# The first MLP of an attention and two-MLP kernel as 48 steps of one tile's up product and another's down share, with one attention unit in a step and the log1p remainder moved to VectorE

## The chip, the cores and the metric

The kernel runs on one core of a Trainium2 chip. A core has TensorE (matmuls, PE in the profile), VectorE (DVE), ScalarE (ACT), GpSimd (POOL) and SyncE (SP, which here only issues transfers), each with an instruction queue of its own that runs in order; they meet at semaphores. The metric is the device time of one execution in microseconds, as the median of several runs.

## What is computed

Window attention (each row sees itself and the 63 before it), then an MLP with a softplus, then four gated experts with a ReLU. All is in float32.

```python
# q, k, v: (2, 8, 576, 64); x becomes (1152, 512) after attention
scores = np.where(mask, scale * q @ k.T, -1e9)           # mask: 0 <= row - col < 64
attn = softmax(scores) @ v
h = x @ w_in                                             # (1152, 2048)
g = np.maximum(h, 0.0) + np.log1p(np.exp(-np.abs(h)))
x = g @ w_out                                            # (1152, 512)
p = domain_probs / (domain_probs.sum(-1, keepdims=True) + 1e-09)
for e in range(4):
    out += p[:, e:e+1] * (np.maximum(x @ w1[e], 0.0) @ w2[e])
```

## The kernel before

**Numbers.** Every float32 operand of the MLPs is split into a high part in float32r and a low part, `wa` (up weights), `wb` (down weights), `xy` (the input) and `hid` (the hidden values) each exist as `[0]` high and `[1]` low, and each product is three matmuls (`TERMS`). So a tile's up product (128 hidden rows by 384 tokens, four k tiles) is 12 matmuls of 128x384, and its down share (four output tiles `t`) is 12 more.

**First MLP.** The 1152 tokens are 3 chunks `c` of 384, the 2048 hidden columns 2 blocks `b` of 8 tiles `f`. A loop over n = 0 to 5 (b = n // 3, c = n % 3) does in each turn 20 stages: eight up products (`up`, L698), then the down products in 12 pieces of 2 or 3 tiles (`down_width`, L713, `PIECES`). Both use the four PSUM banks `ps[0]` to `ps[3]`: up tile f writes bank f % 4, the down sum of output tile t stands in bank t. So up tile f + 4 waits until VectorE has read tile f's bank (`bank_read`), the down sum waits for the last four tiles, and the next turn's up waits for the sums' copies (`down_read`).

**Softplus of a tile.** ScalarE: `absolute` (L381), `exponential` (L386), `logarithm` (L393, log(1+e) into `sp_l`). VectorE: `rounded` (L501, (e + 1) - 1 into `sp_c`), GpSimd: `lost` (L299, e - `sp_c`, the remainder that the logarithm lost), VectorE: `relu_ln` (L507, reads the bank, frees it), `activation` (L515, adds the remainder). Then ScalarE `hidden_high` (L398) and VectorE `hidden_low` (L520) give the two parts of `hid`.

**Attention.** 24 units u of 192 rows by 2 heads, 8 to a chunk. A unit passes `scores` (TensorE L650), `masked_scores` (VectorE L467), `softmax_exp` (ScalarE L349), `row_inverse` (VectorE L474, L476), `normalise` (GpSimd L292), `transpose_probs` (L661), `copy_pT` (ScalarE L358), `weigh_values` (L676), `x_high` (ScalarE L365), `x_low` (VectorE L482). Units 0 to 7 run ahead of the MLP in a prologue of 11 turns j, with the first pieces of up products between them (`STARTS`, `BEFORE`); units 8 to 23 run in the turns n = 0 and 1 behind the stages in `AFTER`. The queries, keys and values of two units are a group g = u // 2, in one of four slots.

**Splits and transfers.** The raw weights come in pairs of tiles into two buffers (`raw_a` up, `raw_b` down). SyncE issues all transfers in one order; the third and later pairs of a block wait until both splits of the pair before the last are done (L213, L214 and L220, L221). In block 0 VectorE makes the high parts (L578, L602) and GpSimd the low ones (L313, L326), at stages given by `UP_SPLIT` and `DOWN_SPLIT`; afterwards ScalarE and VectorE do (L339, L450; L344, L455), except the down weights of block 1, which are VectorE's and GpSimd's too. `first_out` (L528, L530) takes the down sums to `part`, and `y_high` and `y_low` split them for the experts, which start at 286.38 us in the profiled execution (L698 and L728).

## Time and profile before

| | us |
|---|---|
| median of 3 runs (lowest to highest) | 687.87 (685.45 to 688.37) |
| span of the profiled execution | 686.2 |
| TensorE busy | 654.9 |
| VectorE busy | 319.0 |
| ScalarE busy | 224.8 |
| GpSimd busy | 119.4 |
| start of the experts in the profiled execution | 286.38 |

The span is the time from the first to the last instruction of the one execution that was profiled. An engine's busy time is a sum of what its instructions took, in which a wait for a shared resource inside an instruction counts as busy. Matmuls overlap: one takes 0.33 us and the next starts 0.17 us after it, so the pace is read from starts and not from durations.

### The profile page before, as it was taken

How to read it: one execution, taken by the hardware profiler on the slowest of the kernel's cores; microseconds unless marked ns; L12 is line 12 of the kernel's file. 1: busy time of each engine (PE TensorE's matmuls, PEld its weight loads, DVE VectorE, ACT ScalarE, POOL GpSimd, SP SyncE). 2: the span in 40 equal slices, each digit the busy share in tenths (PEclk: the TensorE clock that was granted, in tenths of full speed). 3: DMA queues.
4: the chain of work that ended last, by engine and by line, in shares of the span. 5: the costliest groups of instructions: out<-in, count | busy, mean ns of one | idle time of the engine just before them, and what ended most of it. 6: DMA issues, size and time to landing. Idle time of an engine off the chain costs nothing.

```text
span 686.2 us, 10024 instructions
## 1 busy us (share of the span) xinstructions
PE 654.9 (95%) x3688; PEld 603.9 (88%) x3688; DVE 319.0 (46%) x689; ACT 224.8 (33%) x565; POOL 119.4 (17%) x111
## 2 busy tenths in 40 slices
PE   7886998999969999999999999999999999999998
PEld 6776998898959898998999999898989898989896
DVE  5599369376793939651224232133322142512121
ACT  4655556564531627440112221121311030402020
POOL 3676334231452415000000000000000000000000
PEclk9999999999999999999999999999999999999999
DMA  7662520103030000330003130002120030100101
GB/s 205 195 151 94 138 63 1 51 1 107 22 117 1 0 1 1 123 123 0 1 2 120 22 103 0 1 31 91 47 75 0 0 101 22 61 31 15 38 8 46
DMA packets 39425, 37.94 MB, mean 55 GB/s; under 512 B 12256, under 2 KB 32096, under 8 KB 39392
## 3 DMA queue, kind: packets, MB, share of 16 engines
q1 hardware_dynamic: 39392, 37.51, 18.3%
q8 instruction: 19, 0.31, 0.2%
q14 instruction: 14, 0.11, 0.1%
HBM read 35.15 MB, written 2.36 MB: 55 GB/s over the span
## 4 chain that ended last, share of the span: by engine, by line
PE 71%; DVE 14%; issue 7%; DMA 3%; ACT 2%; SPq 2%; POOL 1%; DVEq 0%; ACTq 0%
PE ps L698 33%; PE ps L728 29%; PE ps L713 6%; DVE sp_l L515 4%; DVE sp_l L507 3%; DVE hid_lo L520 3%; DMA raw_a<-in_w_in 2%; PE ps_o L676 1%; DVE wa_lo L450 1%; SPq L191 1%; DVE prob L467 1%; DVE sp_c L501 1%; ACT prob L349 1%; PE ps_pT L661 1%; ACT sp_l L393 1%
## 5 line engine op out<-in xcount | busy, mean ns | idle before, releaser
L698 PE MATMUL ps<-xy_hi,wa_hi 128*128 128x384 f32 (+1 forms) x576 | 194.2, 337 | 4.5 <-DVE sp_l L507 3.7
L698 PE MATMUL ps<-xy_hi,wa_lo 128*128 128x384 f32 (+1 forms) x576 | 192.8, 335 | 0.0
L698 PE MATMUL ps<-xy_lo,wa_hi 128*128 128x384 f32 (+1 forms) x576 | 192.8, 335 | 0.0
L427 ACT ACTIVATE hid_hi<-ps 128x384 fp32r<-128x384 f32 x96 | 47.3, 492 | 304.1 <-PE ps L698 304.1
L698 PEld LDWEIGHTS ps<-xy_hi,wa_hi 128*128 128x128 f32 x576 | 108.2, 188 | 7.5 <-issue 6.0
L728 PE MATMUL ps<-wb_hi,hid_lo 128*128 128x512 f32 x288 | 112.3, 390 | 0.0
L728 PE MATMUL ps<-wb_lo,hid_hi 128*128 128x512 f32 x288 | 112.2, 390 | 0.0
L728 PE MATMUL ps<-wb_hi,hid_hi 128*128 128x512 f32 x288 | 112.0, 389 | 0.0
L698 PEld LDWEIGHTS ps<-xy_lo,wa_hi 128*128 128x128 f32 x576 | 108.3, 188 | 0.4
L698 PEld LDWEIGHTS ps<-xy_hi,wa_lo 128*128 128x128 f32 x576 | 108.2, 188 | 0.0
L614 DVE SCALAR_TENSOR_TENSOR hid_lo<-ps,hid_hi 128x384 fp32r<-128x384 f32 x96 | 53.5, 558 | 116.0 <-ACT hid_hi L427 116.0
L632 DVE SCALAR_TENSOR_TENSOR part<-ps,gate,part 128x512 f32<-128x512 f32 x36 | 27.0, 751 | 161.0 <-PE ps L728 161.0
L713 PE MATMUL ps<-hid_hi,wb_hi 128*128 128x384 f32 x192 | 68.4, 356 | 14.1 <-DVE sp_l L507 11.5
L299 POOL TENSOR_TENSOR sp_c<-sp_e,sp_c 128x384 f32<-128x384 f32 x48 | 59.9, 1249 | 95.1 <-DVE sp_c L501 95.1
L713 PE MATMUL ps<-hid_hi,wb_lo 128*128 128x384 f32 x192 | 65.0, 339 | 0.0
L713 PE MATMUL ps<-hid_lo,wb_hi 128*128 128x384 f32 x192 | 64.9, 338 | 0.0
L728 PEld LDWEIGHTS ps<-wb_hi,hid_lo 128*128 128x128 f32 x288 | 54.1, 188 | 11.3
L728 PEld LDWEIGHTS ps<-wb_lo,hid_hi 128*128 128x128 f32 x288 | 54.1, 188 | 11.0
L728 PEld LDWEIGHTS ps<-wb_hi,hid_hi 128*128 128x128 f32 x288 | 54.1, 188 | 10.9
L520 DVE TENSOR_TENSOR hid_lo<-sp_l,hid_hi 128x384 fp32r<-128x384 f32 x48 | 57.5, 1197 | 0.0
L713 PEld LDWEIGHTS ps<-hid_hi,wb_hi 128*128 128x128 f32 x192 | 36.3, 189 | 20.7 <-DVE sp_l L507 16.2
L381 ACT ACTIVATE sp_e<-ps 128x384 f32<-128x384 f32 x48 | 23.5, 489 | 55.1 <-PE ps L698 50.7
(74 smaller groups left out, 625.2 us busy)
## 6 DMA issues: line engine op xcount, KB each, us to landing
raw_a<-in_w SPq DMA_DIRECT2D x16, 512.0 KB, 3.8
raw_b<-in_w SPq DMA_DIRECT2D x16, 512.0 KB, 4.0
raw_a<-in_w_in SPq DMA_DIRECT2D x8, 512.0 KB, 5.1
raw_b<-in_w_out SPq DMA_DIRECT2D x8, 512.0 KB, 4.3
v_in<-in_v SPq DMA_DIRECT2D x20, 192.0 KB, 3.6
k_in<-in_kT SPq DMA_DIRECT2D x9, 256.0 KB, 3.5
out_dram<-part SPq DMA_DIRECT2D x9, 256.0 KB, 2.1
q_in<-in_q SPq DMA_DIRECT2D x22, 96.0 KB, 3.0
```

Of the source, the lines that this page charges most:

```text
L191: sp.dma_start(q_slots[s][D * h:D * h + D, :, :, WIN * h:WIN * h + WIN], q[h, :, u, hp0:hp0 + 2, :, :]).then_inc(qk_in[s], 16)
L299: pool.tensor_tensor(sp_c[:, s, :], sp_e[:, s, :], sp_c[:, s, :], ALU.subtract).then_inc(lost_done, 1)
L381: act.activation(sp_e[:, s, :], ps[f % 4][:, 0:CH], ACT.Abs).then_inc(abs_done, 1)
L427: act.activation(hid[0][:, f, :], ps[f % 4][:, 0:CH], ACT.Relu).then_inc(h_hi, 1)
L507: dve.scalar_tensor_tensor(out=l, in0=ps[f % 4][:, 0:CH], scalar=0.0, in1=l, op0=ALU.max, op1=ALU.add).then_inc(bank_read, 1)
L515: dve.tensor_tensor(l, l, sp_c[:, f % 2, :], ALU.add).then_inc(act_done, 1)
L520: dve.tensor_tensor(hid[1][:, f, :], sp_l[:, (i - 1) % 4, :], f32(hid[0][:, f, :]), ALU.subtract).then_inc(h_lo, 1)
L614: dve.scalar_tensor_tensor(out=hid[1][:, f, :], in0=ps[f % 4][:, 0:CH], scalar=0.0, in1=f32(hid[0][:, f, :]), op0=ALU.max, op1=ALU.subtrac ...
L632: dve.scalar_tensor_tensor(out=acc[:, T, :], in0=ps[t][:, :], scalar=gate[:, T, bass.ds(e, 1)], in1=acc[:, T, :], op0=ALU.mult, op1=ALU.ad ...
L698: m = pe.matmul(ps[f % 4][:, 0:CH], wa[a][:, f, k, :], xy[x][:, bass.ds(c, 1), k, :], start=(k == 0 and i == 0), stop=(k == KT - 1 and i = ...
L713: m = pe.matmul(ps[t][:, 0:CH], wb[a][:, f, P * t:P * t + P], hid[x][:, f, :], start=(f == 0 and i == 0), stop=(f == FT - 1 and i == 2))
L728: m = pe.matmul(ps[t][:, :], hid[x][:, f, P * t:P * t + P], wb[a][:, f, :], start=(f == 0 and i == 0), stop=(f == FT - 1 and i == 2))
```

## The change

The turn of 20 stages is gone. The first MLP is now 48 steps k (`STEPS`; n = k // 8, f = k % 8). A step on TensorE is: the up product of tile k; the transposes of unit k + 8; the scores of unit k + 10; the down share of tile k - 3 (`LAG`) for all four output tiles; the weighing of unit k + 8. The last three down shares stand among the first three up products of expert 0.

The eight PSUM banks are divided anew. The down sums have four of their own (`sums`: `ps[2]`, `ps[3]`, `ps_score[1]`, `ps_o`). The up products have `ps[0]` and `ps[1]` in turn up to step 15, and four (`up_banks`) from step 16 on. From unit 8 on all scores go through `ps_score[0]`, and transposed probabilities and outputs share `ps_pT`, so a unit's transposes wait for `x_low` of the unit before it.

`lost` moves from GpSimd to VectorE. The prologue scores units 8 and 9 too (`SCORED` = 10) and weighs 8 as before; of the early pieces of tile 2, none is left. The low parts of block 0's down weights stay on GpSimd, one in each of the steps 0 to 7; those of block 1 go to ScalarE and VectorE (`split_down`). On SyncE the inputs of group 7 move between the third and the fourth pair of down weights.

```diff
+LAG = 3
+STEPS = NB1 * NCH * FT
+N_UNITS = NCH * UPC
+SCORED = 10
+WEIGHED = 8
+        up_banks = [ps[0], ps[1], ps_score[0], ps_pT]
+        sums = [ps[2], ps[3], ps_score[1], ps_o]
+        def up_bank(k):
+            return up_banks[k % 2 if k < N_UNITS - WEIGHED else k % 4]
...
 # SyncE
-            for g in range(5, 7):
-                attention_inputs(g)
-            down_weights(0, down_in(0), (2, 3))
+            attention_inputs(5)
+            attention_inputs(6)
+            down_weights(0, down_in(0), (2,))
+            attention_inputs(7)
+            down_weights(0, down_in(0), (3,))
             up_weights(1, up_in(1), (0, 1))
-            for g in range(7, 12):
+            for g in range(8, 12):
                 attention_inputs(g)
...
 # GpSimd
-                if j < UPC:
+                if j < SCORED:
                     normalise(j)
...
+            for k in range(N_UNITS - SCORED):
+                if k < FT:
+                    pool.wait_ge(wb_hi, k + 1)
+                    pool.tensor_tensor(wb[1][:, k, :], ...)
+                normalise(k + SCORED)
...
 # ScalarE
+            for k in range(STEPS):
+                n, f = k // FT, k % FT
+                absolute(n, f)
+                if k + WEIGHED < N_UNITS:
+                    copy_pT(k + WEIGHED)
+                exponential(n, f)
+                if k > 0:
+                    hidden_high((k - 1) // FT, (k - 1) % FT)
+                logarithm(n, f)
+                if k + SCORED < N_UNITS:
+                    softmax_exp(k + SCORED)
+                if k + WEIGHED < N_UNITS:
+                    x_high(k + WEIGHED)
...
 # VectorE
+            for k in range(STEPS):
+                n, f = k // FT, k % FT
+                if k + SCORED < N_UNITS:
+                    masked_scores(k + SCORED)
+                rounded(n, f)
+                if k > 0:
+                    hidden_low((k - 1) // FT, (k - 1) % FT)
+                lost(n, f)
+                relu_ln(n, f)
+                if k + SCORED < N_UNITS:
+                    row_inverse(k + SCORED)
+                if k + WEIGHED < N_UNITS:
+                    x_low(k + WEIGHED)
+                activation(n, f)
+                if n >= 1 and f == LAG - 1:
+                    for t in range(KT):
+                        first_out(n - 1, t)
+                if n == 0:
+                    dve.wait_ge(raw_b_in[f // 2 % 2], 16 * (f // 4 + 1))
+                    dve.tensor_copy(wb[0][:, f, :], ...).then_inc(wb_hi, 1)
+                if n % NCH == NCH - 1:
+                    split_up(n // NCH + 1, f)
+                if 0 <= k - (NCH - 1) * FT - LAG - 1 < FT:
+                    split_down(1, k - (NCH - 1) * FT - LAG - 1)
...
 # TensorE
-                if j + 1 < UPC:
+                if j + 1 < SCORED:
                     scores(j + 1)
...
+            for s in range(STEPS):
+                n, f = s // FT, s % FT
...
+                up(up_bank(s), f, c, n < NCH, [k for k in range(KT) if n > 0 or (f, k) not in started])
+                if s + WEIGHED < N_UNITS:
+                    transpose_probs(s + WEIGHED)
+                if s + SCORED < N_UNITS:
+                    scores(s + SCORED)
+                if s >= LAG:
+                    down_width((s - LAG) // FT, (s - LAG) % FT)
+                if s + WEIGHED < N_UNITS:
+                    weigh_values(s + WEIGHED)
```

**First place, TensorE in the prologue, turn j = 7.** Before, behind the weighing of unit 3 (the row with `ps<-probT`) come the transposes of unit 5:

```order
L650 MATMUL ps_score<-part 128x128 x3
L661 MATMUL ps_pT<-ident,prob 128x128 x3
L676 MATMUL ps<-probT,v_in 64x64 x6
L661 MATMUL ps<-ident,prob 128x128 x3
L676 MATMUL ps_o<-probT,v_in 64x64 x6
```

Now:

```order
L650 MATMUL ps_score<-part 128x128 x3
L663 MATMUL ps_pT<-ident,prob 128x128 x3
L678 MATMUL ps<-probT,v_in 64x64 x6
L650 MATMUL ps_score<-k_in,q_in 128x128 x3
L663 MATMUL ps<-ident,prob 128x128 x3
L678 MATMUL ps_o<-probT,v_in 64x64 x6
```

The scores of unit 8 have come in ahead of the transposes of unit 5, and those of unit 9 stand in the same way one turn later.

**Second place, VectorE in the turns or steps without attention.** Before, a tile's row of work in the turn n = 2 (`lost` is on GpSimd, between L501 and L515):

```order
L501 TENSOR_SCALAR sp_c<-sp_e 128x384
L515 TENSOR_TENSOR sp_l<-sp_l,sp_c 128x384
L520 TENSOR_TENSOR hid_lo<-sp_l,hid_hi 128x384
L507 SCALAR_TENSOR_TENSOR sp_l<-ps,sp_l 128x384
```

Now, step 19, with one split of up weights:

```order
L490 TENSOR_SCALAR sp_c<-sp_e 128x384
L515 TENSOR_TENSOR hid_lo<-sp_l,hid_hi 128x384
L496 TENSOR_TENSOR sp_c<-sp_e,sp_c 128x384
L502 SCALAR_TENSOR_TENSOR sp_l<-ps_pT,sp_l 128x384
L510 TENSOR_TENSOR sp_l<-sp_l,sp_c 128x384
L450 TENSOR_TENSOR wa_lo<-raw_a,wa_hi 128x512
```

The row with `sp_c<-sp_e,sp_c` is `lost`, and `activation` (`sp_l<-sp_l,sp_c`) has moved from the next tile's turn to the end of its own.

**Third place, SyncE's queue of transfers, from the last pair of block 0's up weights on.** This stretch is the same before and now but for line numbers; here it is as it stands now:

```order
L226 DMA raw_a<-in_w_in 128x4x256
L233 DMA raw_b<-in_w_out 128x2x512 x2
L258 DMA gate<-in_probs 128x9x4
L202 DMA q_in<-in_q 64x6x64 x2
L205 DMA k_in<-in_kT 128x2x256
```

The queries and keys at its end are group 5's, units 10 and 11. What moved is their use: the scores of unit 10 stood in turn n = 0 behind the first down piece, and stand now in step 0.

## Rows read from the trace of the kernel before

**Rows 1.** The page: busy time and share of each engine.
```profile
PE 654.9 (95%) x3688; PEld 603.9 (88%) x3688; DVE 319.0 (46%) x689; ACT 224.8 (33%) x565; POOL 119.4 (17%) x111
```

**Rows 2.** Stretches (us, busy by engine, PEclk, DMA share, GB/s): first MLP.
```profile
216.14:251.18 35.04, 33.85 (x193) 33.21 (x193) 23.45 (x44) 16.06 (x36) 11.24 (x9) 1.00 0.00 1
...
30.60:286.38 255.78, 234.15 (x1477) 221.43 (x1474) 181.32 (x406) 130.15 (x345) 102.89 (x86) 0.99 0.22 63
```

**Rows 3.** The same view, 20 us of attention beside the MLP, and the experts.
```profile
40.00:60.00 20.00, 14.95 (x84) 13.34 (x84) 19.93 (x37) 11.09 (x29) 13.03 (x12) 1.00 0.27 66
...
300.00:686.00 386.00, 382.91 (x1939) 348.44 (x1937) 112.25 (x181) 71.71 (x144) 1.38 (x1) 1.00 0.12 39
```

**Rows 4.** Who waited for whom, TensorE (us in total, times, longest).
```profile
PE ps L713 <- DVE sp_l L507: 11.5, 13, 2.0
```

**Rows 5.** The chain of waits (start us, us, what): TensorE at its pace.
```profile
74.01 0.67 PE ps_score L650 x6
...
77.29 0.67 PE ps_score L650 x6
...
216.14 6.25 PE ps L698 x36
```

**Rows 6.** Timeline (start us, us, instruction, idle): GpSimd and VectorE, 45 us.
```profile
45.38 1.32 POOL L299 TENSOR_TENSOR sp_c<-sp_e,sp_c 128x384 f32<-128x384 f32 x1
...
43.59 0.41 DVE L602 CAST wb_hi<-raw_b 128x512 fp32r<-128x512 f32 x1
...
45.75 1.36 DVE L520 TENSOR_TENSOR hid_lo<-sp_l,hid_hi 128x384 fp32r<-128x384 f32 x1
47.03 0.55 DVE L507 SCALAR_TENSOR_TENSOR sp_l<-ps,sp_l 128x384 f32<-128x384 f32 x1
47.50 0.34 DVE L501 TENSOR_SCALAR sp_c<-sp_e 128x384 f32<-128x384 f32 x1
47.77 0.55 DVE L515 TENSOR_TENSOR sp_l<-sp_l,sp_c 128x384 f32<-128x384 f32 x1
```

**Rows 7.** Groups of equal instructions, VectorE, 0 to 310 us.
```profile
L467 DVE CUSTOM_DVE_ANT_0 prob<-ps_score,mask 128x128 f32<-128x128 f32 x72 | 16.9, 285 | 4.9 <-PE ps_score L650 3.6 <-PE ps L661 0.8 <-PE ps_pT L661 0.6
...
L482 DVE TENSOR_TENSOR xy_lo<-ps_o,xy_hi 128x192 fp32r<-128x192 f32 x21 | 7.5, 357 | 16.8 <-ACT xy_hi L365 16.7
...
L474 DVE TENSOR_SCALAR rowsum<-rowsum 128x3 f32<-128x3 f32 x24 | 5.5, 231 | 13.1 <-ACT prob L349 13.1
```

**Rows 8.** The same for GpSimd and ScalarE.
```profile
L326 POOL TENSOR_TENSOR wb_lo<-raw_b,wb_hi 128x512 fp32r<-128x512 f32 x16 | 21.8, 1367 | 13.0 <-DVE wb_hi L602 13.0
L292 POOL TENSOR_TENSOR prob<-prob,rinv 128x384 f32<-128x384 f32 x24 | 21.0, 873 | 38.5 <-DVE rinv L476 38.5
...
L349 ACT ACTIVATE prob<-prob,negmax 128x128 f32<-128x128 f32 x72 | 28.0, 391 | 19.6 <-DVE negmax L467 19.6
```

**Rows 9.** Timeline of TensorE before the first MLP.
```profile
22.79 0.67 PE L661 MATMUL ps<-ident,prob 128*128 128x128 f32 x3 [1.33 <-POOL prob L292]
23.39 0.91 PE L676 MATMUL ps_o<-probT,v_in 128*64 128x64 f32 x12
```

**Rows 10.** Timeline of the transfer queue of SyncE.
```profile
24.17 0.62 SPq L194 DMA_DIRECT2D k_in<-in_kT  x1
...
29.38 0.37 SPq L215 DMA_DIRECT2D raw_a<-in_w_in  x1
...
34.10 1.78 SPq L194 DMA_DIRECT2D k_in<-in_kT  x1
```

**Rows 11.** Issue to landing of the k transfers issued at 24.17 and at 34.10.
```profile
DMA to landing us min/median/max: 4.4/4.4/4.4
...
DMA to landing us min/median/max: 5.9/5.9/5.9
```

**Rows 12.** Timeline of GpSimd: the split that frees a buffer.
```profile
28.03 1.27 POOL L313 TENSOR_TENSOR wa_lo<-raw_a,wa_hi 128x512 fp32r<-128x512 f32 x1 [0.89 <-DVE wa_hi L578]
```

**Rows 13.** A stretch of 1 us at TensorE's lower clock.
```profile
69.00:70.00 1.00, 1.00 (x4) 1.00 (x4) 0.08 (x1) 1.00 (x6) 0.06 (x1) 0.50 0.62 141
```

More of the change, by code:

```diff
@@ L111, in o_bank @@
         def o_bank(u):
+            if u >= UPC:
+                return ps_pT
             return ps[2] if u < N_ALT and u % 2 else ps_o
@@ new lines, in _ @@
+            for k in range(STEPS):
[17 more added lines that the diff above has]
+                    dve.wait_ge(raw_b_in[f // 2 % 2], 16 * (f // 4 + 1))
+                    dve.tensor_copy(wb[0][:, f, :], raw_b[:, f // 2 % 2, f % 2, :]).then_inc(wb_hi, 1)
+                if n % NCH == NCH - 1:
+                    split_up(n // NCH + 1, f)
+                if 0 <= k - (NCH - 1) * FT - LAG - 1 < FT:
+                    split_down(1, k - (NCH - 1) * FT - LAG - 1)
+                for m in range(NCH, NB1 * NCH):
+                    if 0 <= k - FT * (m + 1) - LAG < KT:
+                        y_low(m, k - FT * (m + 1) - LAG)
+                if k == NCH * FT:
@@ L610, in _ @@
                     gates()
+            hidden_low(NB1 * NCH - 1, FT - 1)
             def relu_low(n, f):
                 dve.wait_ge(h_hi, h_count(n, f))
-                dve.scalar_tensor_tensor(out=hid[1][:, f, :], in0=ps[f % 4][:, 0:CH], scalar=0.0,
+                dve.scalar_tensor_tensor(out=hid[1][:, f, :], in0=up_banks[f % 4][:, 0:CH], scalar=0.0,
                                          in1=f32(hid[0][:, f, :]), op0=ALU.max, op1=ALU.subtract).then_inc(h_lo, 1)
@@ L621, in expert @@
                         relu_low(n, f)
+                        if c == 0 and first and f == LAG - 1:
+                            for t in range(KT):
+                                first_out(NB1 * NCH - 1, t)
                         if c == 0:
@@ L678, in weigh_values, with up @@
                 m.then_inc(pv_done, 1)
[L680 to L686 removed]
             TERMS = ((0, 0), (0, 1), (1, 0))
[L691 removed]
+            def up(bank, f, c, attended=False, ks=range(KT)):
                 for k in ks:
@@ new lines, in _ @@
+                for f, k in STARTS.get(j, ()):
+                    pe.wait_ge(wa_hi, f + 1)
+                    pe.wait_ge(wa_lo, f + 1)
+                    up(up_bank(f), f, 0, True, (k,))
+            for s in range(STEPS):
+                n, f = s // FT, s % FT
+                c = n % NCH
+                if c == 0:
+                    pe.wait_ge(wa_hi, FT * (n // NCH) + f + 1)
+                    pe.wait_ge(wa_lo, FT * (n // NCH) + f + 1)
+                if up_bank(s) is ps_score[0] and up_bank(s - 4) is not ps_score[0]:
+                    pe.wait_ge(negmax_done, N_UNITS)
+                elif up_bank(s) is ps_pT and up_bank(s - 4) is not ps_pT:
+                    pe.wait_ge(x_lo, N_UNITS)
+                elif s >= 2:
+                    pe.wait_ge(bank_read, before_in_bank(s))
+                up(up_bank(s), f, c, n < NCH, [k for k in range(KT) if n > 0 or (f, k) not in started])
[7 more added lines that the diff above has]
+                    weigh_values(s + WEIGHED)
@@ L793, in expert_chunk @@
                     elif first and start:
-                        pe.wait_ge(down_read, KT * 5 + f + 1)
+                        pe.wait_ge(bank_read, STEPS - 4 + f + 1)
                     elif f < TT:
                         pe.wait_ge(down_read, d_count(n - 1, f, True))
-                    up(f, c)
+                    up(up_banks[f % 4], f, c)
+                    if first and start and f < LAG:
+                        down_width(NB1 * NCH - 1, FT - LAG + f)
                 for t in range(TT):
```

210 lines of the change are left out of this document (55 added, 155 removed).

## Prediction

> **What bounds the kernel now.** I read the page first: TensorE is busy 654.9 us of a span of 686.2 [rows 1], so what can be won is in its holes. The stretches say where they are. From 300 us on the experts keep it busy 382.91 of 386 us [rows 3]; I take that part as unchanged. From 30.6 to 286.4 us it is busy 234.15 of 255.78 [rows 2].
>
> Busy time hides part of the loss, so I go by pace. The chain has 36 up matmuls in 6.25 us [rows 5], 0.174 each; a tile's up or down product of 12 takes 2.09 us. One attention unit with 9 down matmuls takes 77.29 - 74.01 = 3.28 us [rows 5], so the unit takes 3.28 - 1.57 = 1.71 us, 0.67 of it its scores. At 30.6 us, 15 of the 1152 matmuls of the first MLP are done; the other 1137 take 197.4 us, 16 units take 27.4 us, together 224.8. The stretch is 255.8 long, so **31 us are lost** there. Nearly all of the largest wait is for `relu_ln` at L507 [rows 4], the read that frees a bank: in the up half of a turn a tile takes VectorE longer than the 2.09 us that TensorE needs. The turn from 216.14 to 251.18 shows this without attention: 35.04 us where the pace asks for 33.4 [rows 2].
>
> Why VectorE is slow stands in the timeline. `hidden_low` takes 1.36 us at 45.75, while GpSimd's `lost` runs from 45.38 to 46.70; a pass of the same size takes 0.55 us at 47.77 [rows 6], where GpSimd is idle. So VectorE's passes with two SBUF inputs wait out a GpSimd pass. From 40 to 60 us it counts as busy 19.93 of 20 us [rows 3], and much of that is this wait.
>
> **The steps at their best.** A step without attention is 24 matmuls, 4.17 us of TensorE. VectorE starts a pass 0.47 us after the one before for a 0.55 us pass and 0.27 us after `rounded` [rows 6]. So five softplus passes take 0.27 + 4 x 0.47 = 2.15 us, and in the steps with both splits (20 to 23) about 1.3 us more, 3.5 in all: under 4.17. `lost` on VectorE adds 0.47 us to a step and is hidden under TensorE; where that cover is gone it costs 0.47 a step. What it removes is the waits of 0.8 us on GpSimd. A tile's chain (abs, exp, `rounded`, `lost`, `relu_ln`, `activation`, high and low part) ends about 9 us after its up product starts, by passes of 0.4 to 0.55 us each and hand-overs; its down share starts 3 x 4.17 + 2.1 = 14.6 us after it. So **the waits on banks and hidden values go** from steps without attention. Next late there is `first_out`: step k's copies of the sums start 3.7 us after the up product's end, the next down share 4.2 us after it, and the first copy takes 0.55, so about 0.2 us are lost at each of five joins (steps 18, 26, 34, 42 and expert 0): 1.0 us. At step 10 attention covers it.
>
> A step with attention is 4.17 + 1.71 = 5.88 us of TensorE. VectorE adds the masked scores (3 x 0.21), `row_inverse` (0.44), `x_low` (0.28) [rows 7], each less the 0.08 us by which passes overlap, and in steps 0 to 7 the high part of a down weight (0.33) [rows 6]: 3.8 us in all. GpSimd's two passes of those steps take 1.3 to 1.37 and 0.87 us [rows 8]; they start behind the high part and hold VectorE's two-input passes for 2.2 us, of which 0.6 is covered by the masked scores, which read PSUM. The round is then 3.8 - 0.63 + 2.3 = 5.4 to 5.5 us. That is under 5.88 by 0.4, so I take TensorE as the bound; the other end is in the rivals.
>
> **The start, which is where most of it is given back.** Two things are wanted sooner than they come.
>
> First, unit 8's scores now stand in turn j = 7 of the prologue, ahead of the transposes of unit 5, which ran at 22.79 us [rows 9]. Unit 8's keys are issued at 24.17 and land 4.4 us later [rows 10, 11], at **28.6 us**. Their issue hangs on splits and units of earlier turns that do not move. So TensorE, in order, waits from 21.5 (the 1.33 us of idle time before 22.79 begin there [rows 9]) to 28.6, and VectorE and ScalarE with it.
>
> From there the chain is: scores 0.9, transposes 0.7, copy and weighing 1.5, the started up piece 1.3 (at half clock, as 0.67 and 0.91 us were at 22.79 and 23.39 [rows 9]), so 32.9; scores of unit 9, transposes and weighing of the next unit with their copy 2.4, so 35.3; `x_high`, then the three exponentials of unit 8 at 0.39 each [rows 8], 36.9; `row_inverse` 0.4, `normalise` of unit 8 0.9 and the low split of up tile 3, 1.3 us and a hand-over: **39.9 us**. That split ended at 29.3 before (28.03 + 1.27) [rows 12], and the transfer of the last pair of up weights left at 29.38 [rows 10].
>
> Second, behind that transfer SyncE has two of down weights, the gates and then group 5 (units 10 and 11), whose scores now stand in step 0. Before, the last pair left at 29.38 and group 5's keys landed at 34.1 + 5.9 = 40.0 [rows 10, 11], 10.6 us later; with the same queue, **39.9 + 10.6 = 50.5 us** for the scores of unit 10. Before, those scores stood behind the first down piece and found their keys.
>
> Then the pipe fills. Steps 0 to 2 have no down share, so the round of VectorE and GpSimd sets them. From the scores of unit 10, `x_low` of unit 8 is done 3.7 us later and that of 9 and 10 each 5.4 us after, which lets the transposes of unit 11 go at 14.6; scores, down share and weighing of step 3 add 3.7. Step 4 starts 18.3 us after the scores, at 68.8. I add 1.0 us for half a clock after the wait: the granted clock was 0.50 from 69 to 70 us [rows 13], behind some microseconds of holes, and a 3.4 us stretch at it costs 1.7. **69.8 us.**
>
> **Other edits.** Group 8's keys stand behind three 0.5 MB transfers that leave when the low part of down tile 3 is done, by the passes about 3.6 us into step 4. With the 10.6 us of the other queue they land 14.2 us into it, and the scores of unit 16 come at 2 x 5.88 + 2.5 = 14.3. With two transfers less in front it is 2 us sooner, with the longest issue later. I take 0 and keep 4 us for the range. The splits of block 1's down weights (step 20 on) may find their transfer 3 us late; six microseconds of slack between `hid` and its use cover it. Reusing `ps_pT` for transposes and outputs costs nothing in full steps: `x_low` is done about 1 us into the next step, the transposes start at 2.1.
>
> **The sum**, against the profiled execution: step 4 starts at 69.8; 44 steps x 4.17 = 183.5; 10 units x 1.71 and 2 without scores x 1.04 = 19.2; joins 1.0; the three last down shares 6.3. The experts' own work then begins at 279.8 where it began at 286.4. The gain is **6.6 us**, the span 679.6. The median of the runs is 1.7 us above the span of the profiled execution, so 681.3.
>
> [...] The trace has VectorE at 19.93 of 20 us [rows 3], and the change gives it one more pass a tile. [...]
>
> **The rivals.**
> *A, the forecast* (54 in 100): TensorE sets the steps, the start is late: 675 to 687.
> *B, the start is cheaper* (16): the chain from 28.6 us overlaps more than I added up, or group 5 comes with less queue before it. If the last pair leaves at 35 instead of 39.9 and the fill takes 14 us, step 4 starts 9 us earlier: 672. For it: much of my chain is hand-overs. Against it: queues run in order.
> *C, VectorE and GpSimd set steps 0 to 7* (15): if none of VectorE's passes overlaps GpSimd's two of 2.24 us, passes count at their full length (0.34 + 4 x 0.55 + 3 x 0.37 + 0.41 + 0.36 + 0.41 = 4.8 us) and four hand-overs cost 0.1 each, a step is 7.5 us instead of 5.88. Then 8 steps cost 12.9 more: 694.2, **slower than before**. It decides from 6.7 us a step on (6.6 / 8 more). For it: 40 to 60 us [rows 3]. Against it: the masked scores and `relu_ln` read PSUM, and showed no such wait.
> *D, the transfers come late again* (15): group 8 lags by as much as group 5's queue did, 4 us, and TensorE runs 2 us more at half clock: 687.5. For it: the k transfer at 34.10 took 1.78 us to issue, where that at 24.17 took 0.62 [rows 10], so a full queue slows the issue too; against it, the time for group 8 above.
> That the start is not late at all would give 665 and has under 3 in 100 (within B): the keys' landing is a fact of the queue.
>
> **How the numbers follow.** The likeliest is A, 681.3. To hold 8 in 10 the range leaves out the lower half of B and the part of C above its own price: 673 to 694. A measurement of this kernel can tell about 0.5% from no change, so faster means under 684.4 and slower above 691.3. Faster: B and most of A, 0.16 + 0.48 = 0.64. Slower: C and a little of D, 0.16. Same: the rest, 0.20.
>
> **What the profile after would show.** TensorE idle from about 21.5 to 28.6 us and again from about 42 to 50, with the scores (L650) waiting for `k_in`: if it isn't, B. Steps of 5.9 us in 4 to 13 by the starts of L691; if 6.7 or more, C. Steps of 4.17 us without attention, with VectorE's two-input passes at 0.55 us; if longer, my account of the wait on GpSimd is wrong. Waits for `part` of a few tenths at the five joins. The experts start at about 280 us. What would make the prediction wrong is above all the length of the two waits in the start, 14 us by this account.

## The result and the profile after

| | before | after |
|---|---|---|
| median (lowest to highest), us | 688.04 (685.45 to 688.37), 4 runs | 681.15 (678.47 to 681.62), 4 runs |
| span of the profiled execution, us | 686.2 | 679.4 |

The ratio is 0.9904, with a 95% interval of 0.9879 to 0.9929: the change takes off about 1%. A second series of the same kernel (`e10_after_again`, below) gave 679.55 us and 0.9892, so a difference of 1.6 us between two kernels says little by itself.

**Busy time.** The page's line on busy time (busy us, share of the span, instructions), against [rows 1]:

```profile
PE 652.8 (96%) x3688; PEld 606.5 (89%) x3688; DVE 306.2 (45%) x737; ACT 227.6 (33%) x573; POOL 47.5 (7%) x55
```

GpSimd has lost 72 us of work. VectorE has 48 passes more (it took 56 from GpSimd and gave 8 to ScalarE) and is nevertheless busy 13 us *less* (319.0 before). Its busy time before was in part waiting. TensorE is busy 2.1 us less, so 4.7 of the 6.8 us by which the span is shorter are idle time of TensorE.

**The stretches** (us, then busy time of TensorE, weight loads, VectorE, ScalarE and GpSimd, granted clock, DMA share, GB/s), against [rows 2, 3]:

```profile
30.00:60.00 30.00, 21.17 (x147) 18.04 (x147) 12.53 (x54) 13.25 (x49) 11.19 (x10) 0.73 0.41 111
...
69.00:270.00 201.00, 200.44 (x1279) 195.07 (x1277) 143.92 (x370) 113.30 (x288) 16.69 (x17) 1.00 0.19 58
```

The kernel after has two parts. From 69 us on TensorE has no hole worth the name: 200.44 of 201 us, where it was busy 234.15 of 255.78 in [rows 2]. Between 30 and 60 us it is busy only 21.17 of 30, and the granted clock there is 0.73, a mean of stretches at 1.00 and at 0.50.

**Who waited for whom**, TensorE (us in total, times, longest), against [rows 4]:

```profile
PE ps_score L650 <- DMA k_in<-in_kT: 15.3, 3, 7.6
PE ps_score L650 <- issue: 2.2, 1, 2.2
```

The 11.5 us for `relu_ln` are gone from the list, and keys that have not landed are in their place. The timeline of TensorE (start us, us, instruction, idle before) shows both places, against [rows 9]:

```profile
22.63 0.57 PE L678 MATMUL ps<-probT,v_in 128*64 128x64 f32 x12
30.11 1.65 PE L650 MATMUL ps_score<-k_in,q_in 128*128 128x128 f32 x6 [6.92 <-DMA k_in<-in_kT]
...
42.63 0.49 PE L663 MATMUL ps_pT<-ident,prob 128*128 128x128 f32 x3
50.71 1.65 PE L650 MATMUL ps_score<-k_in,q_in 128*128 128x128 f32 x6 [7.59 <-DMA k_in<-in_kT]
```

Unit 8's scores wait 6.92 us and unit 10's 7.59. The queue of SyncE says where the keys come from (start us, us the issue took, what):

```profile
25.90 0.62 SPq L205 DMA_DIRECT2D k_in<-in_kT  x1
...
41.15 0.37 SPq L226 DMA_DIRECT2D raw_a<-in_w_in  x1
41.56 1.02 SPq L233 DMA_DIRECT2D raw_b<-in_w_out  x2
42.63 0.47 SPq L258 DMA_DIRECT2D gate<-in_probs  x1
43.14 3.43 SPq L202 DMA_DIRECT2D q_in<-in_q  x2
46.61 1.63 SPq L205 DMA_DIRECT2D k_in<-in_kT  x1
```

(An arrival is not in these rows: the keys issued at 25.90 landed 4.2 us later, those issued at 46.61 after 4.1 us.) The two waits are linked. The last pair of up weights leaves at 41.15 us (29.38 in [rows 10]), because the split that frees its buffer stands behind unit 8 on VectorE and GpSimd. Group 5's keys stand behind that pair in the queue, so the first wait makes the second.

**The steps.** The first up matmuls of steps 4 and 5 in the same timeline of TensorE:

```profile
68.99 0.45 PE L691 MATMUL ps<-xy_hi,wa_hi 128*128 128x384 f32 x1
...
74.89 0.44 PE L691 MATMUL ps<-xy_hi,wa_hi 128*128 128x384 f32 x1
```

From start to start, steps 4 to 13 take 5.90 to 5.92 us each, steps 14 and 15 take 5.24, step 16 takes 4.29, and all later ones 4.16, but for four with 4.56 to 4.58. These hold a join: the place where a token chunk's down sums are copied out before the next chunk's can begin. Expert 0's first up matmul starts at 273.5 us.

### The profile page after: what moved, and what is told of

It is laid out like the page before. It is cut to its first block, busy times and chain, and to the rows that moved or that the text cites. A ratio compares the mean times of both kernels' runs of the same rounds, so it can differ in the third digit from the quotient of the medians.

```text
span 679.4 us, 10005 instructions
## 1 busy us (share of the span) xinstructions
PE 652.8 (96%) x3688; PEld 606.5 (89%) x3688; DVE 306.2 (45%) x737; ACT 227.6 (33%) x573; POOL 47.5 (7%) x55
## 4 chain that ended last, share of the span: by engine, by line
PE 91%; DVE 3%; DMA 2%; SPq 1%; issue 1%; ACT 1%; POOL 1%; DVEq 0%; POOLq 0%
PE ps L691 24%; PE ps L722 19%; PE ps_score L691 10%; PE ps_score L722 10%; PE ps_pT L691 9%; PE ps L707 7%; PE ps_score L707 3%; PE ps_o L707 3%; PE ps_score L650 3%; DMA k_in<-in_kT 2%; PE ps_pT L663 1%; PE ps_pT L678 1%; SPq L202 1%; DVE hid_lo L515 1%; ACT prob L348 1%
## 5 line engine op out<-in xcount | busy, mean ns | idle before, releaser
L691 PE MATMUL ps<-xy_hi,wa_hi 128*128 128x384 f32 (+1 forms) x320 | 110.0, 344 | 0.9 <-DVE xy_lo L482 0.9
L691 PE MATMUL ps<-xy_hi,wa_lo 128*128 128x384 f32 (+1 forms) x320 | 107.8, 337 | 0.0
L691 PE MATMUL ps<-xy_lo,wa_hi 128*128 128x384 f32 (+1 forms) x320 | 107.7, 337 | 0.0
L691 PEld LDWEIGHTS ps<-xy_hi,wa_hi 128*128 128x128 f32 x320 | 60.4, 189 | 3.0 <-issue 1.1
L691 PEld LDWEIGHTS ps<-xy_lo,wa_hi 128*128 128x128 f32 x320 | 60.5, 189 | 0.4
L691 PEld LDWEIGHTS ps<-xy_hi,wa_lo 128*128 128x128 f32 x320 | 60.5, 189 | 0.0
L691 PE MATMUL ps_pT<-xy_hi,wa_lo 128*128 128x384 f32 (+1 forms) x128 | 42.8, 334 | 0.0
L691 PE MATMUL ps_score<-xy_hi,wa_hi 128*128 128x384 f32 (+1 forms) x128 | 42.8, 334 | 0.0
L691 PE MATMUL ps_score<-xy_lo,wa_hi 128*128 128x384 f32 (+1 forms) x128 | 42.8, 334 | 0.0
L691 PE MATMUL ps_score<-xy_hi,wa_lo 128*128 128x384 f32 (+1 forms) x128 | 42.8, 334 | 0.0
```

Source lines behind the costliest of these rows:

```text
L691: m = pe.matmul(bank[:, 0:CH], wa[a][:, f, k, :], xy[x][:, bass.ds(c, 1), k, :], start=(k == 0 and i == 0), stop=(k == KT - 1 and i == 2))
```

## Experiments

All times are medians; ratios are to the kernel before, timed beside each on the same chip. Theory 1 is the prediction's: the new order with `lost` on VectorE takes the holes out, and the start gives most of it back. The first two runs take the two halves of the change apart. The experiments were timed in three groups on three chips (e1 to e4, e5 to e8, e9 and e10), so between groups the ratios are the better comparison.

### The remainder back on GpSimd, in the new order

`e1_lost_gpsimd` is the kernel after with `lost` on GpSimd:

```diff
 # GpSimd
-            for k in range(N_UNITS - SCORED):
+            for k in range(STEPS):
+                lost(k // FT, k % FT)
                 if k < FT:
...
 # VectorE
-                lost(n, f)
```

> The changed kernel with one part undone: the log1p remainder stays on GpSimd, one pass at the head of each of GpSimd's 48 steps. Theory (VectorE's passes with two SBUF inputs wait out a GpSimd pass, but only a round that is near TensorE's 5.9 us feels it): steps without attention stay at 4.2 us, since VectorE's 2.2 us plus about 0.8 us of waiting fit; steps 0 to 7, where GpSimd would have 3.4 us of passes (1.3 + 0.87 + 1.25), go from 5.9 to 6.5 to 7.2 us; the whole 684 to 691. Rival (the new order does it all and the move of the remainder is free either way): 680 to 683, and no step longer.

Measured: **680.11 us** (679.8 to 681.62), ratio 0.9887 [0.9859, 0.9915]; span 677.8. No loss at all, where I had expected 684 to 691; the rival's 680 to 683 is what came. Steps 4 to 13 take 5.91 us and the later ones 4.16, as in the kernel after. The stretch of 30 us in the loaded steps, and GpSimd's group of `lost` passes from 80 to 250 us (busy, mean ns, idle before):

```profile
67.00:97.00 30.00, 30.00 (x230) 28.00 (x230) 18.28 (x72) 18.34 (x64) 17.72 (x17) 1.00 0.54 149
```

```profile
L312 POOL TENSOR_TENSOR sp_c<-sp_e,sp_c 128x384 f32<-128x384 f32 x36 | 48.8, 1356 | 100.0 <-DVE sp_c L498 100.0
```

A pass takes 1356 ns on GpSimd against 552 on VectorE in the kernel after, and TensorE is still busy 30.00 of 30 us. So in the new order the place of `lost` is free. My own theory said that it mattered; it falls here.

### The remainder on VectorE, in the old order

`e2_before_lost_vectore` is the kernel before with that one move, each `lost` at the place in VectorE's row of work at which GpSimd had it:

```diff
 # GpSimd
-                    if 1 <= i < FT + 1:
-                        lost(n, i - 1)
...
 # VectorE
+                    if 1 <= i < FT + 1:
+                        lost(n, i - 1)
```

> The kernel before with that part alone: the remainder on VectorE, order, banks and transfers as before. Theory: in the up halves the wait of 0.8 us in the low-part pass goes and a pass of 0.47 us comes, so a tile there takes VectorE about 2.2 us instead of 2.5, still above TensorE's 2.09; the four bare turns save 1 to 1.5 us each and the two with attention more: 678 to 684 in all. Rival (the remainder's place is worth nothing, the order is everything): 686 to 690.

Measured: **675.11 us** (673.95 to 677.46), ratio 0.9801 [0.9772, 0.9831]. The one move gains 13.5 us, about 6 us more than the whole change, and 3 us more than the best that I expected. Groups of VectorE's passes from 0 to 310 us (busy, mean ns), in the kernel before and then in this run:

```profile
L520 DVE TENSOR_TENSOR hid_lo<-sp_l,hid_hi 128x384 fp32r<-128x384 f32 x48 | 57.5, 1197 | 0.0
```

```profile
L518 DVE TENSOR_TENSOR hid_lo<-sp_l,hid_hi 128x384 fp32r<-128x384 f32 x48 | 28.3, 590 | 0.0
```

`hidden_low` falls from 1197 to 590 ns, 29.2 us in all, and the 48 passes of `lost` add 27.6 us (574 ns each). So they cost VectorE about what it no longer waits. TensorE's waits in its trace, and two stretches of 30 us:

```profile
PE ps L713 <- DVE sp_l L505: 3.9, 6, 1.2
PE ps L713 <- POOL wb_lo L318: 2.7, 4, 1.6
```

```profile
180.00:210.00 30.00, 25.82 (x142) 23.99 (x141) 21.96 (x44) 8.77 (x20) 12.50 (x7) 1.00 0.22 71
210.00:240.00 30.00, 30.00 (x175) 30.00 (x174) 20.27 (x47) 15.84 (x36) 1.39 (x1) 1.00 0.00 1
```

The wait for `relu_ln` falls from 11.5 us [rows 4] to 3.9. From 210 to 240 us TensorE is busy throughout, where the kernel before had holes in a stretch of that kind [rows 2]. The holes left are where weights are split (180 to 210 us). The prediction's cause of the loss is right: VectorE waited out GpSimd's `lost`. Where TensorE pays for it can be seen in a turn without attention. VectorE's round for one tile takes 2.49 us in the kernel before (`rounded` starts at 226.33 and at 228.82 us) and 2.13 in this run (220.89 and 223.02), where TensorE makes a tile in 2.08. In the up half TensorE still runs at its pace, 96 matmuls in 16.6 us in both, since four banks give it room. The first down products need the banks of the last four tiles, and there it waits, 0.53 us at 236.43 and then, in TensorE's timeline of the kernel before:

```profile
238.93 0.44 PE L713 MATMUL ps<-hid_hi,wb_hi 128*128 128x384 f32 x1 [0.66 <-DVE sp_l L507]
```

In this run a turn of that kind (208.76 to 242.04 us) has no such wait and takes 33.3 us instead of 35.0. The six turns together, from the first up product to the experts, take 242.0 us (33.80 to 275.83) where they took 255.8: 13.8 us less.

What the prediction missed is that each half of the change removes this loss alone. In the old order VectorE has to keep up with a tile every 2.08 us, so its round counts; in the new order a step of 4.16 or 5.91 us brings one tile, and VectorE's round fits with `lost` on either engine. The gains don't add.

### Is it GpSimd that would set the loaded steps?

Rival C had a step of 7.5 us because GpSimd's passes hold up VectorE. `e8_gpsimd_load` is `e1_lost_gpsimd` with one more 128x512 GpSimd pass in each of steps 0 to 15; its output isn't used.

```diff
                 lost(k // FT, k % FT)
+                if k < 2 * FT:
+                    pool.wait_ge(extra, k + 1)
+                    pool.tensor_tensor(part[:, 2, 512:1024], part[:, 2, 0:512],
+                                       part[:, 2, 0:512], ALU.subtract).then_inc(extra, 1)
```

> The changed kernel with the remainder on GpSimd, as in the first run, and one more GpSimd pass of 128x512 with both inputs in SBUF in each of steps 0 to 15, whose result is not used: 4.7 us of GpSimd passes in steps 0 to 7 and 3.4 in 8 to 15. Theory 1 (the two engines exclude each other in every pass of VectorE with two SBUF inputs, 1.5 us a step with the high part and the rounding): steps 0 to 7 take 6.2 to 6.8 us, steps 8 to 13 stay at 5.9, the whole 683 to 690. Theory 2 (they overlap far more than that, as the first run suggests, where 3.4 us cost nothing): all steps stay at 5.91, the whole 680 to 682.

Measured: **681.51 us** (679.68 to 682.63), ratio 0.9907 [0.988, 0.9933]; every loaded step is still 5.91 us. The same 30 us and one of VectorE's passes in its timeline:

```profile
67.00:97.00 30.00, 30.00 (x230) 28.25 (x230) 21.75 (x74) 18.38 (x63) 23.92 (x22) 1.00 0.53 146
```

```profile
87.22 1.06 DVE L487 TENSOR_SCALAR rowsum<-rowsum 128x3 f32<-128x3 f32 x1 [0.37 <-ACT prob L361]
...
90.84 0.29 DVE L480 CUSTOM_DVE_ANT_0 prob<-ps_score,mask 128x128 f32<-128x128 f32 x1 [1.30 <-PE ps_score L656]
```

With GpSimd busy 23.92 of 30 us (17.72 in `e1_lost_gpsimd`), VectorE's busy time grows by 3.5 us without any more work (over the same five steps, 21.04 against 17.58 us for 73 instructions): a pass over 128x3 takes 1.06 us instead of 0.24 in the step before it, and `activation` takes 1.02 us at 76.46, where GpSimd's additional pass runs from 76.03 to 77.07, against 0.55 at 88.66, where no GpSimd pass runs. But VectorE still has 1.2 to 1.8 us of idle time in front of a unit's masked scores, in which it waits for TensorE. The second theory of this run, 680 to 682 us, is what came. Rival C is out, and not by little.

### The start: two transfers moved

Two edits each move one late input. `e3_group4_own_slot` gives group 4 (units 8 and 9) buffers of its own in the part of `part` that is idle at this time, so that its transfers wait for no unit, and puts the third pair of up weights behind them:

```diff
+        SLOT = 12 * P + 2 * (UNIT + WIN)
...
+            early[:, SLOT * i:SLOT * i + 6 * P].rearrange("p (t w c) -> p t w c", t=2, w=3) for i in range(2)]
...
-            return g if g <= SLOTS else g % SLOTS
+            return g if g <= SLOTS + 1 else g % SLOTS
...
-                if g > SLOTS:
+                if g > SLOTS + 1:
...
-            up_weights(0, up_in(0), (2,))
...
+            up_weights(0, up_in(0), (2,))
```

> The changed kernel with group 4 (units 8 and 9) in a fifth slot of its own, so that its queries, keys and values are issued ahead of the third pair of up weights and wait for no unit. Theory (the scores of unit 8 hold TensorE's queue for the keys, and all that follows is late by this): the wait of about 7 us at 23 us goes, the last pair of up weights leaves 8 to 10 us sooner, group 5 and step 4 come 6 to 10 us sooner: 671 to 676. Rival (the start is set by VectorE's and ScalarE's chain and the wait lies beside it): 679 to 682.

Measured: **676.4 us** (675.7 to 679.83), ratio 0.984 [0.9802, 0.9878]; span 674.4. TensorE's largest wait:

```profile
PE ps_score L654 <- DMA k_in<-in_kT: 8.9, 2, 8.3
```

The wait of 6.9 us for group 4 is gone. The last pair of up weights leaves at 35.5 us instead of 41.2, group 5's keys land at 45.8, and step 4 starts at 64.1. All moved by about 5 us, less than the 6 to 10 I had expected: TensorE reaches the second wait earlier and waits longer there, 8.3 us.

`e4_group5_first` puts group 5 ahead of that last pair instead:

```diff
+            attention_inputs(5)
...
-            attention_inputs(5)
```

> The changed kernel with group 5's transfers ahead of the last pair of up weights, the first down weights and the gates. Theory (the second wait, 7.6 us before the scores of unit 10, is the queue in front of its keys): that wait goes, but VectorE still stands at the high parts of up tiles 6 and 7 until the last pair lands near 45 us, so step 4 comes 4 to 7 us sooner: 674 to 678. Rival (the wait for the last pair of up weights takes its whole place): 680 to 683.

Measured: **676.62 us** (675.42 to 677.58), ratio 0.9826 [0.9797, 0.9854]; step 4 starts at 65.0. The scores of unit 10 start at 42.67 us without a wait. The late weights take its place, in VectorE's timeline and then in TensorE's:

```profile
45.71 0.76 DVE L573 CAST wa_hi<-raw_a 128x512 fp32r<-128x512 f32 x2 [3.41 <-DMA raw_a<-in_w_in]
```

```profile
PE ps_score L650 <- DMA k_in<-in_kT: 7.8, 2, 7.0
PE ps_pT L663 <- DVE xy_lo L482: 5.3, 2, 5.1
```

VectorE stands 3.41 us before the splits of up tiles 6 and 7, which come in its order ahead of unit 10, and TensorE waits 5.1 us for it. This is the forecast of the theory; the rival's 680 to 683 would have needed a longer wait.

`e5_both` has both edits:

> The changed kernel with group 4 in a slot of its own and group 5's transfers ahead of the last pair of up weights, both together. Each alone left the other's wait standing (step 4 at 64.1 and 65.0 us instead of 69.0). Theory (the start is one chain of late inputs and nothing else): no scores wait for k_in for more than 1 us; what is left is VectorE's wait for the last pair of up weights, near 39 us, so step 4 starts at 57 to 60 us, the whole 668 to 672. Rival (the prologue of ten scored units is itself as long as this): step 4 not before 63 us, 674 or more.

Measured: **670.63 us** (669.23 to 672.59), ratio 0.9755 [0.9727, 0.9784]; step 4 starts at 58.6. Here the gains add, 4.75 + 4.53 = 9.3 us of the 10.5 measured, since they take away two different waits. No scores wait more than 0.5 us for their keys. The largest wait left is again VectorE's for the last pair of up weights, 3.78 us, which TensorE sees as:

```profile
PE ps_pT L667 <- DVE xy_lo L485: 5.8, 2, 5.5
```

`e7_start` takes that one away too: the splits of up tiles 6 and 7 move to the ends of steps 0 and 1, those of the down tiles to two steps later, and on SyncE groups 7 and 8 each stand ahead of a pair of down weights:

```diff
-        UP_SPLIT = {3: (0,), 4: (1,), 6: (2,), 8: (3,), 9: (4,), 10: (5, 6, 7)}
+        UP_SPLIT = {3: (0,), 4: (1,), 6: (2,), 8: (3,), 9: (4,), 10: (5,)}
...
-            down_weights(0, down_in(0), (2,))
             attention_inputs(7)
-            down_weights(0, down_in(0), (3,))
+            down_weights(0, down_in(0), (2,))
+            attention_inputs(8)
             up_weights(1, up_in(1), (0, 1))
-            for g in range(8, 12):
+            down_weights(0, down_in(0), (3,))
+            for g in range(9, 12):
...
 # VectorE
-                if n == 0:
+                if k < 2:
+                    u = 6 + k
+                    dve.wait_ge(raw_a_in[u // 2 % 2], 16 * (u // 4 + 1))
+                    dve.tensor_copy(wa[0][:, u, :, :], ...).then_inc(wa_hi, 1)
+                elif k < FT + 2:
+                    d = k - 2
...
 # GpSimd
-                if k < FT:
+                if k < 2:
+                    u = 6 + k
...
+                elif k < FT + 2:
+                    d = k - 2
...
```

> As the run with both input moves, and further: the splits of up tiles 6 and 7 stand at the ends of steps 0 and 1 instead of ahead of step 0, the splits of down tile f at the end of step f + 2 instead of f, and groups 7 and 8 leave before the third and the fourth pair of down weights. Theory (steps 0 to 2 are set by VectorE's round with GpSimd, and by the wait for the last pair of up weights in front of it): step 4 starts 2 to 4 us sooner than with the two input moves alone, 665 to 670. Rival (TensorE's own work and the attention chain set it by then): within 1 us of that run.

Measured: **665.35 us** (664.02 to 667.73), ratio 0.9676 [0.9644, 0.9708]; the fastest kernel of this study, 2.3% below the kernel after. Step 4 starts at 54.4, 4.2 us sooner than in `e5_both`, and the steps behind it are unchanged, 5.9 and 4.16 us. In steps 1 to 3 TensorE still waits 1.23, 1.17 and 0.93 us for `x_low`, and here for a down split:

```profile
50.05 0.41 PE L723 MATMUL ps<-hid_hi,wb_hi 128*128 128x384 f32 x1 [0.96 <-POOL wb_lo L335]
```

From 50.4 to 53.8 us the matmuls start 0.32 us apart instead of 0.17, and the granted clock is 0.50.

### The place of the remainder once more, with the start mended

`e9_start_lost_gpsimd` is `e7_start` with `lost` back on GpSimd (the edit of `e1_lost_gpsimd`), and `e10_after_again` is the kernel after itself beside it.

> The kernel e7_start (start mended, 665.35 us) with the remainder of log1p back on GpSimd, as in e1_lost_gpsimd. Theory 1, the remainder's engine costs nothing where the later tiles of a step cover the chain, and the seven joins between token chunks lose 0.28 us instead of 0.41 each: 664 to 666 us, ratio to e7_start within 0.3%. Rival, with the start mended the steps 0 to 7 have splits of up and down weights on both engines and GpSimd's longer queue delays the split of a down weight (TensorE already waited 0.96 us for one at 50 us in e7_start): 667 to 671 us, with the wait for the split of a down weight grown to 3 us or more.

> The changed kernel itself, as it is, beside e9 on the same chip, so that the place of the remainder can be compared in both orders against runs of the same call. Theory 1 (the place is free in the new order): 679.5 to 682.5 us, within 0.3% of the 680.11 us of e1_lost_gpsimd. Rival (the remainder on VectorE costs the 0.13 us more at each of the joins and a little in the start): 681.5 to 683 us, and e1_lost_gpsimd clearly below it.

Measured: `e9_start_lost_gpsimd` **668.8 us** (667.71 to 669.51), ratio 0.9732 [0.9709, 0.9755]; `e10_after_again` **679.55 us** (678.55 to 681.75), ratio 0.9892 [0.9868, 0.9916]. The second is as theory 1 says: 679.55 and 681.15 us for `lost` on VectorE, 680.11 for it on GpSimd. (The joins are four, not seven as the first expectation has it.) The first misses theory 1's 664 to 666 us. It has the rival's number (3.4 us above `e7_start`) but not its mechanism: the wait for the split of a down weight is 0.96 us in both. The traces part earlier. In `e9_start_lost_gpsimd`, and then in `e7_start`:

```profile
25.03 1.62 PE L667 MATMUL ps_score<-part 128*128 128x128 f32 x6 [3.04 <-issue]
```

```profile
23.57 0.91 PE L666 MATMUL ps_score<-part 128*128 128x128 f32 x6 [1.46 <-issue]
```

These are the scores of unit 8, 1.5 us later and at half clock (1.62 us instead of 0.91), in the prologue, where no remainder is computed and the two kernels do the same work. The rows name no releaser, but the record of the transfers does: group 4's keys are issued at 16.41 us in both runs and land 8.5 us later in `e9_start_lost_gpsimd`, at 24.9, and 7.1 us later in `e7_start`, at 23.5. The first up matmul is 2.8 us later; by step 4 it is 1.5 us, since this run has no half clock at 50 us, and from there on `e9_start_lost_gpsimd` gains 0.13 us at each join. The profiled spans are 0.9 us apart (665.5 and 664.6), less than the medians. So in these two traces it is a transfer ahead of the MLP that makes the difference, and not the remainder. Why it landed later is open, and whether it explains the whole 3.4 us of the medians too: the two were not run on the same chip.

### Two steps back instead of three

`e6_lag2` takes the down share two steps back:

```diff
-LAG = 3
+LAG = 2
```

> The changed kernel with the down share 2 steps behind its up product instead of 3. Theory (a tile's chain ends about 9 us after its up product starts, and at 2 steps the down share starts 10.4 us after it): steps stay at 4.16 and 5.91 us, joins no longer than 0.5 us, the whole within 1.5 us of the 681 of the changed kernel. Rival (the chain is longer than its passes add up to, and the third step of lag is needed): steps without attention of 4.5 us or more with TensorE waiting for hid_lo, 690 or more.

Measured: **684.75 us** (684.07 to 686.42), ratio 0.9956 [0.9937, 0.9975], 3.6 us above the kernel after; my theory allowed 1.5, the rival wanted 9. The steps are 5.91 and 4.16 us but for one, step 21, which takes 9.98. The loss is there, in TensorE's timeline and in ScalarE's:

```profile
161.29 0.34 PE L691 MATMUL ps<-xy_hi,wa_lo 128*128 128x384 f32 x1
165.64 0.46 PE L707 MATMUL ps<-hid_hi,wb_hi 128*128 128x384 f32 x1 [4.01 <-DVE hid_lo L515]
```

```profile
162.92 0.63 ACT L343 ACTIVATE wb_hi<-raw_b 128x512 fp32r<-128x512 f32 x1 [7.18 <-DMA raw_b<-in_w_out]
```

ScalarE waits 7.18 us for block 1's down weights, and the tile it was working on comes late. TensorE stands idle for 4.0 us, and then its 12 down matmuls start 0.32 us apart, at half clock, which is 1.6 us more: 5.8 us in all. The whole kernel loses less, since at step 4 (68.4 us, against 69.0) it had already done one down share of 2.1 us more. In `e10_after_again`, the kernel after once more, step 4 starts at 66.4 us, so a lead of this size in the start says nothing of the lag. In the kernel after, the same instruction waits 2.97 us, in ScalarE's timeline:

```profile
163.42 0.63 ACT L343 ACTIVATE wb_hi<-raw_b 128x512 fp32r<-128x512 f32 x1 [2.97 <-DMA raw_b<-in_w_out]
```

The weights land at the same time in both (163 us); with a lag of 2 they are asked for one step earlier and there is one step less of slack behind them. The third step of lag pays for this transfer, and in the other steps it buys nothing.

## Why the prediction was right

The number was right (681.3 against 681.15, span 679.6 against 679.4), and so were nearly all of its steps; three sizes were off and cancelled. That it agrees to 0.2 us is luck: the four runs lie between 678.47 and 681.62, and in the trace of `e10_after_again`, the same kernel, step 4 starts at 66.4 us instead of 69.0 and the span is 676.9.

- **What is lost and why: right.** `e2_before_lost_vectore` shows the cause by itself: `hidden_low` at 590 ns instead of 1197, and the turns of the first MLP together 13.8 of the 31 us shorter that the prediction had as lost.
- **TensorE sets the steps: right.** 4.17 and 5.88 us forecast, 4.16 and 5.91 measured; steps 14 and 15, forecast at 4.17 + 1.04, took 5.24. The 0.4 us of margin that I gave VectorE and GpSimd in steps 0 to 7 was mis-sized. I took 3.8 us of VectorE's own work plus 2.3 of waiting on GpSimd. In VectorE's and GpSimd's timelines (start us, us, instruction, idle) of a step with both:

```profile
82.02 0.42 DVE L595 CAST wb_hi<-raw_b 128x512 fp32r<-128x512 f32 x1
84.21 0.29 DVE L467 CUSTOM_DVE_ANT_0 prob<-ps_score,mask 128x128 f32<-128x128 f32 x1 [1.77 <-PE ps_score L650]
```

```profile
82.52 1.28 POOL L325 TENSOR_TENSOR wb_lo<-raw_b,wb_hi 128x512 fp32r<-128x512 f32 x1 [3.85 <-DVE wb_hi L595]
83.76 0.83 POOL L305 TENSOR_TENSOR prob<-prob,rinv 128x384 f32<-128x384 f32 x1
```

  GpSimd's two passes run from 82.5 to 84.6 us, and VectorE is idle from 82.4 to 84.2, since it has to wait for the scores. GpSimd's passes fall into a wait that is there anyway, so they add nothing to the step. The real margin is about 1.8 us a step, and rival C deserved far less than 15 in 100.
- **The waits in the start: right in place, cause and length.** Forecast from 21.5 to 28.6 us and from about 42 to 50.5; measured 23.2 to 30.1 and 43.1 to 50.7. The prologue was 1.7 us later than in the trace of before: group 4's keys were issued at 25.90, not 24.17. In `e10_after_again` they were issued at 23.14, so this is no effect of the change. The last up pair left at 41.15, forecast 39.9, also 1.3 later. Group 5's keys then landed 9.6 us behind it (10.6 forecast), though the two query transfers took 3.43 us to issue.
- **The fill: right by two errors.** Step 4 starts at 69.0, forecast 69.8. The fill took 18.3 us from the scores (50.7), as forecast with 18.3, but part of that is half clock that I had counted beside it as 1.0 us.
- **The joins: mis-sized.** 0.2 us each forecast; TensorE's timeline has one here:

```profile
153.11 0.34 PE L691 MATMUL ps_pT<-xy_hi,wa_lo 128*128 128x384 f32 x1
153.59 0.41 PE L707 MATMUL ps<-hid_hi,wb_hi 128*128 128x384 f32 x1
```

  The first down matmul starts 0.48 us behind the last up matmul instead of 0.17, and the step is 0.41 longer. With `lost` on GpSimd (`e1_lost_gpsimd`) it is 0.28: VectorE has one pass less ahead of the copies but waits 0.45 us for GpSimd's, and the copies come 0.13 us earlier in the step. That is 1.6 us for four joins (at the fifth, in expert 0, the starts of the up products show none) where the forecast had 1.0 for five; with 5.91 for 5.88 in ten steps this cancelled the 0.8 us of the start. Expert 0's first up product, at 273.5 us, is on the forecast to a tenth (69.8 + 183.5 + 19.2 + 1.0).
- **Group 8, and block 1's down weights: right.** There is no third wait for keys behind 50.71 us. The prediction had group 8's keys land 0.1 us ahead of their use, by the 10.6 us of the other queue; they landed at 80.7 us, 8.4 us behind the first of the transfers ahead of them, and were used at 83.3. The last section has what made group 5's queue the slower one. The down weights are 2.97 us late where the prediction had 3, covered as it said; `e6_lag2` shows the cover being used up.
- **One more pass for a busy engine: right.** VectorE at 19.93 of 20 us [rows 3] took one more pass per tile in the old order, and the kernel got 13.5 us faster (`e2_before_lost_vectore`): part of that busy time was waiting. A VectorE pass with two SBUF inputs took longer beside a GpSimd pass: `hidden_low` 1197 ns with `lost` on GpSimd and 590 with it on VectorE, `activation` 1.02 us beside the additional pass of `e8_gpsimd_load` and 0.55 where no GpSimd pass ran. How far the wait reaches shows in [rows 6]: `hidden_low`, begun at 45.75 us beside `lost`, ends at 47.11, 0.41 us behind the end of `lost`. The pass of 0.55 us at 47.77, where the prediction has GpSimd idle, is not quite alone: the next `lost` begins at 47.92, and the pass, begun 0.15 us ahead of it, is not held. In `e1_lost_gpsimd` and `e8_gpsimd_load` GpSimd's passes, 17.72 and 23.92 of 30 us, cost the kernel nothing, with loaded steps of 5.91 us in both, since VectorE has slack there.
- **A slip in the rivals.** D's price of 4 us and 2 us on 681.3 is 687.3, not 687.5; nothing hangs on it.

What the prediction did not see is that a change can have two remedies for one loss in it. It put the whole gain of the first MLP down to the move of `lost` plus the order, and never asked what either would give alone. `e2_before_lost_vectore` keeps the old start and gets 13.5 us for an edit of a few lines; the new order gets rid of the same waits, but asks for units 8 and 10 earlier than their inputs come, and gives back some 16 us. Only with its start mended does it lead (665.35 against 675.11).

## What to carry to other kernels

When a change has two parts that act on the same wait, price each alone before the sum: here one of them was free and the other cost the start. When a pipeline is deepened, look at what it now wants first, and put the transfers in the order of first use; a late input that stands in front of another in a queue makes the next one late as well (5 us for each edit alone, 10.5 for both, 16 with the splits moved). And ask of an engine's long passes whether it has idle time in the same step: here a wait inside VectorE's idle time of 1.2 to 1.8 us a step cost nothing.

## What the runs showed of the hardware

**In these traces half clock follows waits, and lasts.** I had counted 1.0 us for it, with a stretch of 3.4 us as in the kernel before, where the granted clock was 0.50 from 67.44 to 70.86 us. The kernel after has three stretches at 0.50, two of them of some 10 us, here as windows (columns as above):

```profile
12.40:19.10 6.70, 6.10 (x43) 5.24 (x43) 1.93 (x12) 2.48 (x10) 1.65 (x2) 0.50 1.03 268
26.10:36.10 10.00, 5.99 (x33) 5.46 (x33) 1.43 (x9) 1.97 (x8) 2.07 (x3) 0.50 0.38 97
46.60:56.60 10.00, 5.89 (x31) 5.27 (x32) 3.41 (x14) 2.44 (x10) 2.09 (x3) 0.50 0.79 188
```

Two of them begin inside the two waits for keys and end 6 us behind them, and hold some 6 us of busy time each, which is up to 3 us of loss per stretch if all of it was on the path. In the timeline a unit's scores take 1.65 us at 30.11 and 0.83 at 71.51. `e6_lag2` has the plainest case: TensorE runs at full clock for 90 us, is idle for 4.0 us, and the 12 matmuls behind the wait start 0.32 us apart. The mean granted clock follows the order of the kernels: 0.98 to 0.987 in the runs of the kernel after, 0.987 to 0.990 with both transfers moved, 0.994 to 1.0 with the splits moved too (0.990 to 0.995 in `e9_start_lost_gpsimd`). So a wait can cost more than its length: the one of 4.0 us in `e6_lag2` made its step 5.8 us longer. Between runs of one kernel these stretches come and go, and the time goes with them: 676.9 us of span at a mean clock of 0.987 in `e10_after_again`, 679.4 at 0.98 here.

**Some issues on SyncE are long, and the queue's length does not explain it.** The two query transfers ahead of group 5's keys took 3.43 us to issue and the keys 1.63, where the keys' issue at 25.90 took 0.62. The prediction (rival D) put such an issue down to the full queue, three 0.5 MB transfers. But group 8's inputs, later in the same trace, stand behind three 0.5 MB transfers too, issued in the 1.5 us before:

```profile
72.30 0.37 SPq L233 DMA_DIRECT2D raw_b<-in_w_out  x1
72.78 0.96 SPq L226 DMA_DIRECT2D raw_a<-in_w_in  x2
73.79 1.29 SPq L202 DMA_DIRECT2D q_in<-in_q  x2
75.13 0.61 SPq L205 DMA_DIRECT2D k_in<-in_kT  x1
```

What group 5 has right in front of it, and group 8 has not, is the transfer of the gates (`gate`, 18 KB, in the trace 1152 packets of 16 bytes that landed 6.6 us after the issue). In `e4_group5_first`, where group 5 is issued ahead of it and group 6 behind it, the long issues are group 6's:

```profile
36.64 1.26 SPq L202 DMA_DIRECT2D q_in<-in_q  x2
37.95 0.61 SPq L205 DMA_DIRECT2D k_in<-in_kT  x1
...
42.33 0.52 SPq L259 DMA_DIRECT2D gate<-in_probs  x1
42.89 3.58 SPq L202 DMA_DIRECT2D q_in<-in_q  x2
46.52 1.89 SPq L205 DMA_DIRECT2D k_in<-in_kT  x1
```

All twelve traces show the same: the longest issues of queries (2.58 to 4.65 us for two) and of keys (1.63 to 2.98 us) are those right behind the gates; elsewhere two queries take at most 2.06 us. It costs group 5's keys about 3.2 us here (3.43 + 1.63 instead of 1.29 + 0.61). The gates are first used at step 24. No run moved their transfer alone, so neither the cause nor the gain of moving it is shown.
